# Spreading the weight product and the weight preparation of a three-part transformer kernel over its first linear attention and first batch

## The reference, cut to what matters

```python
kv = einsum('bhsd,bhse->bhde', k, v);  out = einsum('bhsd,bhde->bhse', q, kv)
x = out / sqrt(mean(out * out, -1) + 1e-06) * g_norm        # 8 heads side by side: 512 columns
for e in range(4):                                          # top 2 of 4 by x @ w_gate
    q, k, v = x @ wq[e], x @ wk[e], x @ wv[e]
    ye = softmax(causal(q @ k.T / 8)) @ v @ wo[e]
    y += gate[:, e] * ye
h = gelu_tanh(y @ w_in);  u, v = h[..., :512], h[..., 512:]
v_s = einsum('ts,bsd->btd', w_sg, layernorm(v) * g_ln) + b_sg[:, None]
result = y + (u * v_s) @ w_out
```

## Time and profile before

| | us |
|---|---|
| median of 3 runs | 925.42 |
| lowest and highest | 923.89, 925.64 |
| profiled execution | 923.37 |
| its span | 921.6 |
| PE busy in the span | 889.8 (97%) |
| DVE busy | 460.2 (50%) |
| ACT busy | 410.9 (45%) |
| POOL busy | 176.3 (19%) |

### The profile page before, as it was taken

The page is one execution under the profiler, slowest core; times in us unless marked ns, Lnnn a source line. Parts: engine busy times, 40 slices in busy tenths (PEclk is TensorE's granted clock), DMA queues, the critical chain, the costliest instruction groups (busy, mean ns, idle before and its releaser), DMA issues.

```text
span 921.6 us, 17530 instructions
## 1 busy us (share of the span) xinstructions
PE 889.8 (97%) x7009; PEld 765.3 (83%) x7009; DVE 460.2 (50%) x1218; ACT 410.9 (45%) x971; POOL 176.3 (19%) x209
## 2 busy tenths in 40 slices
PE   7699999999999999999999999999999999999897
PEld 3587898979888798978989789897988879897796
DVE  1667623475345743377334762347534574337730
ACT  0646523473335633365244652347333563336521
POOL 0400233003320033101330023300332003310230
DMA  9930303003030032100230030300303000000001
GB/s 278 268 62 2 97 8 94 10 2 104 6 98 2 1 104 60 44 2 22 84 87 18 1 101 4 95 9 2 104 7 97 2 2 1 20 33 1 1 1 52
DMA packets 77648, 45.76 MB, mean 50 GB/s; under 512 B 54592, under 2 KB 70976, under 8 KB 77568
## 3 DMA queue, kind: packets, MB, share of 16 engines
q1 hardware_dynamic: 77568, 44.63, 18.4%
HBM read 35.19 MB, written 9.44 MB: 48 GB/s over the span
## 4 chain that ended last, share of the span: by engine, by line
PE 81%; DVE 10%; ACT 7%; issue 1%; POOL 0%; DMA 0%; POOLq 0%; ACTq 0%; DVEq 0%
PE w L871 38%; PE t L871 19%; ACT probs L566 5%; PE t L925 4%; PE t L1013 4%; PE w L910 3%; DVE neg_max L686 3%; PE w L1058 3%; DVE probs L707 2%; PE t L941 2%; PE t L1002 2%; PE t L957 2%; PE w L978 2%; PE t L1021 2%; ACT work L579 1%; DVE yT L812 1%
## 5 line engine op out<-in xcount | busy, mean ns | idle before, releaser
L871 PE MATMUL w<-wout_s,big 128*128 128x512 f32 x480 | 119.2, 397 | 1.6 <-DVE big L735 1.6
L871 PE MATMUL w<-wsgT_s,big 128*128 128x288 f32 x768 | 110.8, 300 | 0.0
L871 PE MATMUL t<-big,wqk_s 128*128 128x288 f32 x768 | 109.6, 298 | 0.0
L871 PEld LDWEIGHTS w<-wsgT_s,big 128*128 128x128 f32 x768 | 103.3, 189 | 5.2 <-issue 5.2
L871 PEld LDWEIGHTS w<-wout_s,big 128*128 128x128 f32 x480 | 89.3, 188 | 22.0 <-DVE big L735 2.1
L871 PEld LDWEIGHTS t<-big,wqk_s 128*128 128x128 f32 x768 | 102.8, 188 | 0.4
L566 ACT ACTIVATE probs<-w,neg_max 128x64 f32<-128x64 f32 (+4 forms) x160 | 83.0, 525 | 44.5 <-DVE neg_max L686 44.5
L487 POOL TENSOR_TENSOR var_eps<-bn,eps_t 128x1 f32<-128x1 f32 x40 | 13.3, 333 | 445.6 <-DVE bn L723 444.9
L579 ACT ACTIVATE work<-t 128x384 f32<-128x384 f32 (+3 forms) x160 | 63.1, 448 | 44.5 <-PE t L925 44.1
L837 DVE SCALAR_TENSOR_TENSOR work<-w,gln_c,bias_t 128x576 f32<-128x576 f32 x32 | 26.2, 818 | 111.7 <-PE w L871 111.7
L600 ACT ACTIVATE big<-work 128x576 fp32r<-128x576 f32 x32 | 21.9, 686 | 133.1 <-POOL work L494 133.1
(11 more groups left out here) (104 smaller groups left out, 1417.2 us busy)
## 6 DMA issues: line engine op xcount, KB each, us to landing
kin<-in_k_dram SPq DMA_DIRECT2D x8, 1024.0 KB, 6.4
vin<-in_v_dram SPq DMA_DIRECT2D x8, 1024.0 KB, 9.5
qin<-in_q_dram SPq DMA_DIRECT2D x32, 256.0 KB, 4.8
out_dram<-work SPq DMA_DIRECT2D x32, 256.0 KB, 2.1
staged_win<-in_moe_w_in_dram SPq DMA_DIRECT2D x4, 512.0 KB, 5.7
probs<-in_moe_w_sg_dram SPq DMA_DIRECT2D x4, 288.0 KB, 4.1
kin<-in_k_dram SPq DMA_DIRECT2D x8, 128.0 KB, 3.2
vin<-in_v_dram SPq DMA_DIRECT2D x8, 128.0 KB, 7.4
```

The lines of the kernel that those rows point to most:

```text
L871: last = nc.tensor.matmul(o, stationary(hs, c), mv(hm, c), start=c == of[0] and p == 0, stop=c == of[-1] and p == len(PASSES) - 1)
```

## The change

FIRST is written in another order: the key-value product, the q transposes and the first o units come after two of the four chunks of the weight product, and chunks 2 and 3 stand behind o 2 and o 3 (the chunks keep their size). The split of wo stands ahead of w2 3, that of wqk and wv behind x 2 and x 3. The transposes of w_sg and the split of w_out leave FIRST and are spread over steps 1 to 7 of batch 0's attention (table LATE): w_sg in five units of 4 transposes (128x512) and one unit wsgR of 5 narrow ones (128x320), w_out in four units of 128x512. The w_sg units now take slots of the ring. The staging places change with it (w_sg in `staged` and `vin`, w_out in `kin`), two chunks of w_in are loaded behind q, w_sg and what follows wait for the key-value product, and k and v of batch 1 are loaded when the last of w_out is prepared. The loop's bookkeeping (Slots, count) is written for batches unrolled by number. Batches 1 to 7 have the same units in the same order.

```diff
-    FIRST = [("woT", 0), ("woT", 1)] + [("w2", c) for c in range(DC)] + [("split", "wo")]
-    FIRST += [("kv", c) for c in range(DC)] + [("qT", 0), ("qT", 1), ("o", 0), ("qT", 2), ("qT", 3), ("o", 1),
-              ("split", "wqk"), ("qT", 4), ("o", 2), ("split", "wv"), ("x", 0), ("o", 3), ("double", 0), ("x", 1), ("o", 4),
-              ("x", 2), ("wsgT", 0), ("wsgT", 1), ("x", 3), ("wsgT", 2), ("wsgT", 3), ("x", 4), ("wsgT", 4), ("split", "wout")]
-    PREPARED = [("w2", c) for c in range(EP)] + [x for x in FIRST if x[0] in ("split", "wsgT")]
+    FIRST = [("woT", 0), ("woT", 1), ("w2", 0), ("w2", 1)] + [("kv", c) for c in range(DC)]
+    FIRST += [("qT", 0), ("qT", 1), ("o", 0), ("qT", 2), ("qT", 3), ("o", 1), ("qT", 4), ("o", 2), ("w2", 2), ("x", 0),
+              ("o", 3), ("split", "wo"), ("w2", 3), ("x", 1), ("o", 4), ("x", 2), ("split", "wqk"), ("x", 3),
+              ("split", "wv"), ("x", 4)]
+    LATE = {1: [("double", 0), ("wsgT", 0)], 2: [("wsgT", 1)], 3: [("wsgT", 2)], 4: [("wsgT", 3), ("wout", 0)],
+            5: [("wsgT", 4), ("wout", 1)], 6: [("wsgR", 0), ("wout", 2)], 7: [("wout", 3)]}
...
-        ATTENTION += BETWEEN.get(n, []) + [("pv", n - 3)] * (n >= 3)
+            plan += BETWEEN.get(n, []) + late.get(n, []) + [("pv", n - 3)] * (n >= 3)
...
+    PLAN = {-1: FIRST, 0: attention(LATE) + MLP + MIXED}
+    PREPARED = [("w2", c) for c in range(EP)]
+    PREPARED += [x for part in (-1, 0) for x in PLAN[part] if x[0] in ("split", "wsgT", "wsgR", "wout")]
...
-            elif kind in ("u", "vs", "woT", "wsgT"):
+            elif kind in ("u", "vs", "woT"):
...
-            elif kind in ("v", "h") or (kind == "qk" and j[1] == 1):
+            elif kind in ("v", "h", "wsgT", "wsgR") or (kind == "qk" and j[1] == 1):
...
-            for c in range(DC):
-                sp.dma_start(win_st[c], w_in[P * c:P * (c + 1), :]).then_inc(w_loaded[f"win_{c}"], 16)
+            load_win((0, 1))
             load_kv(0)
             load_q(0)
+            load_win((2, 3))
...
+            u.wait_full(sp, -1, ("kv", 0))
             for t in range(4):
                 sp.dma_start(wsg_st[t][:, PAD:SP], w_sg[P * t:P * (t + 1), :]).then_inc(w_loaded["wsg"], 16)
...
+            u.wait_full(sp, 0, ("wsgR", 0))
+            sp.wait_ge(w_lo, 3 + FC)
             load_kv(1)
...
-            pe.wait_ge(w_lo, 3)
-            for i in range(B - 1):
-                body("loop", i, (i, 0), (i, 1))
+            pe.wait_ge(w_lo, 3)
+            for part in range(B):
+                body(part)
```

317 lines of the change are left out of this document (161 added, 156 removed).

## The result

| | before | after |
|---|---|---|
| median of 6 runs each, same chip | 924.68 | 934.51 |
| lowest and highest | 923.05, 926.20 | 930.67, 936.90 |
| profiled execution | 923.37 | 934.18 |
| its span | 921.6 | 932.4 |

The ratio is 1.0103, with a 95% interval of 1.0076 to 1.0129: the change makes the kernel slower by 1.0% (7 to 12 us). The forecast was 932.7 us, within 925.5 to 936.5; two of the six times of the changed kernel (936.86 and 936.90) lie above that range, the median inside it. A second measurement of the same kernel, on another chip, gave 932.87 us (932.36 to 933.24), ratio 1.0089 (1.0071 to 1.0107).

A forecast was written before the change was run, and what follows sets the result against it. It took the kernel as bound by a chain of waits, 81% TensorE's, touchable only in the front and batch 0's attention. -1.2 + 6.5 + 2.0 = +7.3 us gave 932.7 us on the 925.42 median, range 925.5 to 936.5.

The forecast's parts named there:

- 116 to 118 named as a sign: Batch 0's first attention product to batch 1's: forecast to take 116 to 118 us, against 109.7 before.
- Term 1: Front, up to the key-value product: it starts at 16.9 us and the chain stands 7.6 us earlier.
- Term 2: Front, from the key-value product to attention's first product: most is given back, start at 49.2 instead of 50.41 us.
- the walk: Step-by-step timing of the new order through the front and batch 0's attention, using durations of the old profile.
- gain of 1.2: Start of batch 0's attention: forecast 1.2 us earlier, at 49.2 instead of 50.41 us.
- Term 3: Batch 0's attention: the w_sg and w_out work added there costs 6.5 us, within bounds of 2.7 and 12.7.
- Rival C: Batch 0's attention: late work hides, only TensorE's 2.7 us is paid; 926.9 or 928.9 us by clock; chance 0.14.
- Term 4: End of the front into attention: idle gaps drop TensorE's clock, costing 2.0 us, bounded by 0 and 3.
- Rival B: Start of attention: TensorE's clock stays up, so the change costs +5.3 us, 930.7 us; chance 0.23.
- Rival D: Front: moved blocks and low parts fit idle time, attention starts at 42, total -3.8 us, 921.6; chance 0.10.
- covers costed at nothing: Later loads of batch 1's k and v (covered by some 4 us), w_sg and w_out: no cost.
- sum of 7.3 us: Whole kernel: forecast total change, -1.2 + 6.5 + 2.0 = +7.3 us.

The follow-up runs named there:

- after_again: The changed kernel itself, unedited, measured and profiled a second time on another chip: 932.87 us, ratio 1.0089.
- e1_wait: Changed kernel with VectorE's cast waits in ScalarE's order, so wo's low part waits for its own cast only: 931.05 us, ratio 1.0065.
- e2_front: Changed kernel with the w_sg transposes and w_out split put back into the front, keeping the new front order: 932.18 us, ratio 1.0077.
- e5_busy: Changed kernel plus extra TensorE products with unused results in the front's idle stretches: 933.32 us, ratio 1.0094.
- e11_fill: Changed kernel with whole weight product first, own-cast waits, late work in steps 0 to 3, five filler products: 924.47 us; without fillers 926.51.

## Why the prediction was right

The time, the sign and the mechanism held: a shorter start of the front that is given back inside it, and late work that the chain of batch 0 pays. The distance from the first product of attention to that of batch 1 is 117.5 us (53.50 to 171.02), in the 116 to 118 named as a sign. By its own steps:

**Term 1.** The key-value product was forecast at 16.9 and came at 16.71 and 16.91. The landing of v (14.3) was wrong: in after the last v load was issued at 5.1 and took 11.6 us, so 16.7, in after_again 4.4 + 10.6 = 15.0. It cost next to nothing, as the product was due at 16.7 anyway. The last part of q was put at 19.7 and landed at 22.2 and 20.3. The step that failed is taking a whole 2.7 us off by the bytes that are no longer ahead. q's last load was issued only 0.3 and 2.0 us earlier than before (each issue of a q load holds SyncE for 1.1 to 2.8 us), and the rate from 5 to 10 us was 328 and 350 GB/s instead of the 384 of the earlier trace rows.

**Term 2.** The wait of wo's low part for three casts is in the trace (2.67 us, ended by the cast at 40.04), with the order of things behind it as walked. In after_again each mark comes 0.4 to 1.1 us later than in the walk: wo at 37.92 for 37.0, the first product at 50.33 for 49.2. In the first execution the first product is 4.3 later: 2.7 us is q, some 1.2 the lower clock at the q transposes and the first o (1.92 and 1.89 us for eight, 1.06 and 1.13 in after_again), and 0.4 the walk's own shortfall, as in after_again. I had looked for a fall of the clock only at the end of the front; the wait for q, which the change uncovers by moving TensorE's work away from it, is another. So the "gain of 1.2" was +3.1 in one execution and -0.1 in the other. The wait itself is worth 2.3 us of the start by e1_wait (14.83 for 17.10 us behind the last chunk), so the start hung on it as the walk had it.

**Term 3** was right in size and nearly in its parts. The exponentials on ScalarE mark each step; before, then after (steps 4, 5, 7 and 8):

```profile
74.79 0.53 ACT L566 ACTIVATE probs<-w,neg_max 128x320 f32<-128x320 f32 x1
...
77.17 0.53 ACT L566 ACTIVATE probs<-w,neg_max 128x320 f32<-128x320 f32 x1 [0.36 <-DVE neg_max L686]
...
82.55 0.64 ACT L566 ACTIVATE probs<-w,neg_max 128x448 f32<-128x448 f32 x1 [0.19 <-DVE neg_max L686]
...
87.53 0.74 ACT L566 ACTIVATE probs<-w,neg_max 128x576 f32<-128x576 f32 x1 [1.53 <-DVE neg_max L686]
```

```profile
81.81 0.53 ACT L563 ACTIVATE probs<-w,neg_max 128x320 f32<-128x320 f32 x1
...
85.61 0.53 ACT L563 ACTIVATE probs<-w,neg_max 128x320 f32<-128x320 f32 x1 [0.83 <-DVE neg_max L678]
...
93.09 0.64 ACT L563 ACTIVATE probs<-w,neg_max 128x448 f32<-128x448 f32 x1 [0.67 <-DVE neg_max L678]
...
98.49 0.74 ACT L563 ACTIVATE probs<-w,neg_max 128x576 f32<-128x576 f32 x1 [1.60 <-DVE neg_max L678]
```

Less the 4.4 us of the later start and the first 48 products, the shifts are 2.6, 4.0, 6.1 and 6.5 us. The walk had 2.1 at step 4, 3.7 at step 5, 5.8 at step 7 and 6.5 at step 8. What it named as the cause is there; step 4 on VectorE, after:

```profile
83.47 0.69 DVE L763 TENSOR_TENSOR wsgT_s<-t,wsgT_s 128x512 fp32r<-128x512 f32 x1 [0.82 <-ACT wsgT_s L522]
...
84.08 0.68 DVE L772 TENSOR_TENSOR wout_s<-kin,wout_s 128x512 fp32r<-128x512 f32 x1
...
84.67 0.42 DVE L813 TENSOR_TENSOR yT<-t,yT 128x256 fp32r<-128x256 f32 x1
```

Both low parts stand ahead of yT's, which waits 1.2 us behind the first of them. The chain that ended last holds these units too, between the start of attention and the u product: 4.65 us of them on VectorE, 2.46 on ScalarE and 1.08 on TensorE, 8.2 together, for a stretch that is 6.5 longer. One of its pieces:

```profile
76.65 0.69 DVE wsgT_s L763
```

Rival C, that VectorE's and ScalarE's idle shares hide this, is refuted by the 6.5 us of six profiles, against 0.0 in e2_front, which has the weight product in the same chunks and no late work.

**Term 4** was 2.0 and is 1.4 at the first products, in the place and for the reason given: idle stretches of 4.2, 2.5 and 3.1 us with transposes between. Rival B (the clock stays up) fell; by e5_busy and e11_fill the idle time is the cause. The term's size depends on the front: 1.2 to 2.4 us in the kernels without fillers.

**Rival D** (faster) needed attention to start by 44; it started at 50.3 or later. The covers costed at nothing held: neither the later load of batch 1's k and v nor those of w_sg and w_out appear as a wait in the chain after. The sum of 7.3 us stands against 7.8 (after_again) and 10.95 (after) at the u product. The medians differ by 9.8: the forecast of the time was 1.8 us too low and that of the change 2.5, as the kernel before came 0.7 under its earlier median. What was missing is q's landing and the clock behind it, of which the first traced execution has much and the second little; how many of the six had them, and so how much luck there is in the median's place inside the range, no trace shows.

## What to carry to other kernels

Work that looks free in an engine's idle quarter is paid for when that idle time is the engine waiting inside a serial chain (6.5 us here); put it where the chain is not yet formed (4.6) or leave it where it filled gaps. Moving a block out of the way of a later step also uncovers whatever the block had covered: here the landing of q, and TensorE's clock, which the old w_sg transposes had kept up. A mark compared between two executions needs a check of what lies ahead of it: a gain of 0.6 us at the start of attention was one of 2.3 from the last mark that the edit does not touch. When a preparation unit changes the kind of buffer that it uses, its old place in the order may be closed to it.
